# Who weighs the first token tiles, one operation for a tile's parts, an earlier first tile of a group, and four buffers for the last results

## The chip, the cores and the metric

The kernel runs on one core of a Trainium2 chip. The metric is the device time of one launch, in microseconds. The trace is one execution of the same program, taken by the hardware profiler.

## The reference

```python
q, k, v: (2, 8, 768, 64)
k_sum, v_sum = k, v by blocks of 32 rows: max, mean          # 24 per head
scores = [q k^T / 8 within a window of 16 | q k_sum^T / 8 + log 32]
x = softmax(scores) @ [v | v_sum]                            # -> (1536, 512)

noisy = x @ w_gate + log1p(exp(x @ w_noise)) * noise         # 8 experts
two best experts per token, weights = softmax of their two logits
x = sum over the two: weight * (relu(x @ w1[e]) @ w2[e])     # w1 512x1024, w2 1024x512

h = x @ w_in                                                 # 512 x 2048
out = max(0.01 h, h) @ w_out                                 # 2048 x 512
```

The change touches the last two lines and the sum over the two experts ahead of them.

## The kernel before

Three stages follow each other: attention with the gate and the sorting by expert (to 140 us), the experts (to 529 us), and the last two products, called the last stage here. Every fp32 product is made of three: both operands are split into a high part in fp32r, and a low part, what is left. For `a @ w` TensorE adds `a_hi w_hi + a_lo w_hi + a_hi w_lo`. ScalarE makes the high parts of what TensorE put out, VectorE the low parts. Each engine has its own program, and its instructions run in the order in which they are written. The engines meet at semaphores (`wait_ge`, `then_inc`).

**Picking and weighing.** The experts' outputs lie in DRAM, sorted by expert (`y_by_tile`). The 1536 tokens are 12 tiles of 128 (`NT`), in three groups (`FG`) of four (`TW`). For each tile GpSimd gathers two sets of rows, `a` and `b`, by indirect DMA (L664). Tiles 0 and 1 and all later ones land in `y_pick` (two buffers, by parity), tiles 2 and 3 in the weight buffer `stage`. Weighing makes `a = w0 a + w1 b`. GpSimd does it for tiles 0 and 1 (`combine_early`, `EARLY = 2`, three operations), VectorE for all others (`combine`, two operations, L1096 and L1098). The semaphore `combined` counts weighed tiles.

**Turning.** `turn_tokens(i, m)` on TensorE transposes tile m of group i, four 128x128 blocks, into one of two PSUM banks `f_xT_bank[m % 2]` (L1430). ScalarE's `xT_part` copies it to `f_xT_hi` in four operations of 128x128 (L822), and VectorE's `f_xT_out` makes `f_xT_lo` in four (L1105). A transpose waits until the low part of the tile two before it is done, since that frees the bank.

**Products.** The 2048 hidden features are 16 chunks (`FC`) of 128. `f_first(i, c)` makes chunk c of `h` for the group's 512 tokens: 12 matmuls of 512 columns (L1443 to L1445) into `f_h_bank[c % 2]`. Then `chunk`: ScalarE copies it (L830), VectorE takes the leaky maximum (L1113), ScalarE makes the high part (L834) and VectorE the low part (L1115). `f_second(i, c)` adds chunk c's share to the four results of the group, in four PSUM banks `f_y_bank` (L1458 to L1460), 12 matmuls. TensorE alternates `f_first(c)` and `f_second(c - 1)`. The tiles of group i + 1 are turned in the second half of group i's chunks, one ahead of every second chunk.

**Start of the stage.** For group 0 TensorE turns tiles 0 to 3. After tiles 2 and 3 it does chunks 0 and 1 for the first 256 tokens, later the other 256 tokens of each. The weights of chunks 8 to 15 come last: once all four tiles are turned, SP loads them into `stage` in eight pieces, and ScalarE (L838) and VectorE (L1131) split two of them after each of chunks 1 to 4.

**Group borders.** VectorE weighs tile 0 of the next group at the top of its loop over i, after `chunk(i, 7)`, and TensorE turns it before `f_first(i, 8)`. `group_out` copies the four results of a group to `f_y`, which has two buffers, and SP stores each (L445). The third copy waits until the store of the first has landed, also for the last group, whose copies end the kernel.

The other names: `KD` = 4, `KF` = 8 and `GT` = 512; `p01`, `p23`, `p45` and `p67` are PSUM tensors of two banks each; `xT_bank` and `y_bank` of the expert stage are in `p45` and `p67`.

Of the kernel before, what the change touches and what calls it, by code (L numbers as in the profile page):

```python
# [55 lines left out]
EARLY = 2  # L56
# [13 lines left out]
def build(nc, q, k, v, w_gate, w_noise, noise, w1, w2, w_in, w_out, out):  # L70
    ctx = ExitStack()
    with ctx:
# [148 lines left out]
        f_y_done = sem("f_y_done"); f_y_ready = sem("f_y_ready"); out_stored = [sem(f"out_stored{i}") for i in range(2)]  # L221

# [21 lines left out]
        f_xT_bank = [p23[:, DM * i:DM * (i + 1)] for i in range(2)]  # L244
        f_y_bank = [(p45, p67)[m // 2][:, DM * (m % 2):DM * (m % 2 + 1)] for m in range(TW)]
# [46 lines left out]
        def _(sp):  # L292
# [149 lines left out]
            with sp.Fori(0, NT // 2) as j:  # L442
                for r in range(2):
                    sp.wait_ge(f_y_ready, 2 * j + r + 1)
                    sp.dma_start(out[bass.ds((2 * j + r) * P, P), :], f_y[:, r, :]).then_inc(out_stored[r], 16)  # L445
            for r in range(2):
                sp.wait_ge(out_stored[r], 16 * (NT // 2 + 1))
# [3 lines left out]
        def _(pool):  # L451
# [205 lines left out]
            for i in range(NT):  # L657
                if i == TW:
                    for m in range(EARLY):
                        combine_early(m)  # L660
                if i >= TW:
                    pool.wait_ge(f_x_turned, i - 1)
                for kk in range(2):
                    pool.indirect_dma_start(out=pick_of(i, i % TW)[kk], out_offset=None, in_=ys_dram,  # L664
                                            in_offset=bass.IndirectOffsetOnAxis(ap=slots[:, kk, i:i + 1], axis=0)).then_inc(
                                                first_picked[i] if i < TW else picked[i % 2], 16)
# [3 lines left out]
        def _(act):  # L670
# [148 lines left out]
            def xT_part(i, m, par):  # L819
                act.wait_ge(f_x_turned, TW * i + m + 1)  # L820
                for c in range(KD):
                    last = nc.scalar.copy(f_xT_hi[:, group_columns(par, c, m * P, P)], f_xT_bank[m % 2][:, c * P:(c + 1) * P])  # L822
                last.then_inc(f_xT_hi_ready, 1)
# [30 lines left out]
            for c in range(KF, FC):  # L854
                chunk(FG - 1, c)


        @block.vector
        def _(dve):
# [228 lines left out]
            def combine(i, m):  # L1088

                t = TW * i + m  # L1090
                a, b = pick_of(t, m)
                if is_later(t, TW):
                    dve.wait_ge(picked[m % 2], 16 * (t - TW - m % 2 + 2))
                else:
                    dve.wait_ge(first_picked[m], 32)
                nc.vector.tensor_scalar(a, a, top_w[:, 0, bass.ds(t, 1)], None, ALU.mult).then_inc(first_term, 1)  # L1096
                dve.wait_ge(first_term, t - EARLY + 1)
                nc.vector.scalar_tensor_tensor(out=a, in0=b, scalar=top_w[:, 1, bass.ds(t, 1)], in1=a,  # L1098
                                               op0=ALU.mult, op1=ALU.add).then_inc(combined, 1)

            def f_xT_out(i, m, par):
                dve.wait_ge(f_xT_hi_ready, TW * i + m + 1)
                for c in range(KD):
                    cols = group_columns(par, c, m * P, P)
                    last = nc.vector.tensor_tensor(f_xT_lo[:, cols], f_xT_bank[m % 2][:, c * P:(c + 1) * P], f_xT_hi[:, cols].bitcast(F32), ALU.subtract)  # L1105
                last.then_inc(f_xT_lo_ready, 1)
# [10 lines left out]
            def group_out(i, first=False):  # L1117
                if first:
                    dve.wait_ge(y_stored, 16 * TILES)
# [13 lines left out]
            dve.wait_ge(combined, EARLY)  # L1133
            for m in range(EARLY, TW):
                combine(0, m)
                f_xT_out(0, m - EARLY, 0)
            for m in range(EARLY, TW):
                f_xT_out(0, m, 0)
            for c in range(KF):
                chunk(0, c)  # L1140
                for piece in last_pieces[c]:
                    last_piece(piece)
            with dve.Fori(1, FG) as i:
                combine(i, 0)
                for c in range(KF, FC):
                    m = (c - KF) // 2
                    if c % 2 == 0:
                        f_xT_out(i, m, i * -1 + 2)
# [4 lines left out]
                group_out(i - 1, True)  # L1153
                for c in range(1, KF):
                    chunk(i, c)
            for c in range(KF, FC):
                chunk(FG - 1, c)
            group_out(FG - 1)
# [3 lines left out]
        def _(pe):  # L1162
# [261 lines left out]
            def turn_tokens(i, m):  # L1424
                t = TW * i + m
                pe.wait_ge(combined, t + 1)
                if is_later(t, 2):
                    pe.wait_ge(f_xT_lo_ready, t - 1)
                for c in range(KD):
                    last = nc.tensor.transpose(f_xT_bank[m % 2][:, c * P:(c + 1) * P], pick_of(t, m)[0][:, c * P:(c + 1) * P], ident[:])  # L1430
# [35 lines left out]
            for m in range(TW):  # L1466
                turn_tokens(0, m)
                if m >= TW // 2:
                    pe.wait_ge(w1_ready, HALF_A + 1)
                    pe.wait_ge(f_xT_lo_ready, TW // 2)  # L1470
                    f_first(0, m - TW // 2, 0, 0, GT // 2)
            pe.wait_ge(f_xT_lo_ready, TW)
            for c in range(KF):
                f_first(0, c, 0, *((GT // 2, GT // 2) if c < 2 else ()))
                if c == 0:
                    pe.wait_ge(w2_ready, HALF_A + 1)
                else:
                    f_second(0, c - 1)
# [31 lines left out]
```

## Time and profile before

| | us |
|---|---|
| median of 3 runs | 812.42 (811.93 to 812.96) |
| the profiled execution | 813.08 |
| its span, first to last instruction | 811.5 |
| TensorE busy with matmuls | 771.6 (95%) |
| VectorE busy | 272.5 (34%) |
| ScalarE busy | 239.5 (30%) |
| GpSimd busy | 370.3 (46%) |
| TensorE's mean granted clock | 0.984 of full speed |

Times in the trace count from the first instruction. A row in order of time gives the start, the duration, the engine, the line of the kernel and the operation, and in brackets how long the engine had been idle and what ended this. Matmuls overlap: each lasts 0.39 us with 512 columns, while the next starts 0.23 us later. So TensorE's pace is read from start to start. PE is TensorE, DVE VectorE, ACT ScalarE, POOL GpSimd and SP the engine that issues most loads and stores.

### The profile page before, as it was taken

Reading aid. Unit: us, or ns where it says so; the run is one execution under the profiler, and the core shown is the slowest. Engines: PE = TensorE matmul, PEld = TensorE weight load, DVE = VectorE, ACT = ScalarE, POOL = GpSimd, SP = SyncE. Lnnn points to the kernel's source line nnn. Section 1 sums busy time; section 2 is a strip of 40 time slices with the busy share of each in tenths; the row PEclk is TensorE's granted clock in tenths of the full one; section 3 lists DMA queues with packets and bytes.
Section 4 is the critical chain, followed back from the end, with each engine's and each line's share of the span. In section 5 each row is a group of like instructions: output and inputs, shape, how many; then the busy total and the mean of one; then the engine's idle time right before and its main releaser. Section 6 shows DMA issues by size and latency. Waiting matters only on the chain.

```text
span 811.5 us, 12513 instructions
## 1 busy us (share of the span) xinstructions
PE 771.6 (95%) x4092; PEld 638.0 (79%) x4093; DVE 272.5 (34%) x521; ACT 239.5 (30%) x429; POOL 370.3 (46%) x317
## 2 busy tenths in 40 slices
PE   5998988799999999999999999979999999999997
PEld 4887865588888888888888888868788887888885
DVE  3776656022212212212212212256343324332223
ACT  3787555121121122122112112135232222322221
POOL 5586932568888686938478771510010001000000
PEclk9999879899999999999999999999999999999999
DMA  9959764995353625234352721353010101010001
GB/s 199 217 132 234 198 222 156 318 331 188 111 193 103 214 90 207 90 142 155 130 168 93 243 78 44 112 171 102 26 53 27 53 0 52 0 52 0 1 1 52
DMA packets 77891, 100.54 MB, mean 124 GB/s; under 512 B 46452, under 2 KB 49524, under 8 KB 77492
## 3 DMA queue, kind: packets, MB, share of 16 engines
q1 hardware_dynamic: 60164, 48.71, 21.9%
q0 software_dynamic: 12464, 43.79, 16.7%
q10 hardware_dynamic: 5232, 7.64, 2.5%
q8 instruction: 18, 0.29, 0.1%
q14 instruction: 13, 0.11, 0.0%
HBM read 78.27 MB, written 23.68 MB: 126 GB/s over the span
## 4 chain that ended last, share of the span: by engine, by line
PE 84%; DMA 4%; POOL 3%; DVE 3%; SPq 3%; issue 2%; ACT 1%; DVEq 0%; POOLq 0%; ACTq 0%
PE p L1353 42%; PE p L1443 5%; PE p L1445 5%; PE p L1444 5%; PE p L1458 5%; PE p L1460 5%; PE p L1459 5%; PE p L1345 3%; POOL stage L502 2%; PE p L1340 2%; DMA qk_other<-in_q 1%; DMA mean_rows<-v_means 1%; PE p L1308 1%; PE p L1252 1%; SPq L295 1%
## 5 line engine op out<-in xcount | busy, mean ns | idle before, releaser
L550 POOL TENSOR_TENSOR w_lo<-stage,w_hi 128x1024 fp32r<-128x1024 f32 x56 | 134.0, 2394 | 4.7
L1353 PE MATMUL p<-w_hi,xT_hi 128*128 x248 | 99.8, 402 | 1.7 <-issue 1.7
L664 POOL DMA_INDIRECT y_pick<-y_by_tile,slots x20 | 19.1, 957 | 172.5 <-PE p L1430 147.6
L1353 PE MATMUL p<-w_hi,xT_lo 128*128 x248 | 97.1, 392 | 0.0
L1353 PE MATMUL p<-w_lo,xT_hi 128*128 x248 | 97.0, 391 | 0.0
L1353 PE MATMUL p<-w_hi,hT_hi 128*128 x240 | 96.6, 402 | 0.0
L1353 PE MATMUL p<-w_lo,hT_hi 128*128 x240 | 93.9, 391 | 0.0
L1353 PE MATMUL p<-w_hi,hT_lo 128*128 x240 | 93.5, 390 | 0.0
L1443 PE MATMUL p<-f_xT_hi,w_hi 128*128 (+2 forms) x200 | 77.2, 386 | 1.7 <-DVE f_xT_lo L1105 1.7
L798 ACT CAST hT_hi<-p 128x1024 fp32r<-128x1024 f32 x30 | 30.4, 1014 | 158.0 <-PE p L1345 144.7
L1458 PE MATMUL p<-w_hi,f_hT_hi 128*128 128x512 f32 x192 | 74.9, 390 | 1.4 <-DVE f_hT_lo L1115 1.3
L1445 PE MATMUL p<-f_xT_hi,w_lo 128*128 (+2 forms) x200 | 76.2, 381 | 0.0
L1444 PE MATMUL p<-f_xT_lo,w_hi 128*128 (+2 forms) x200 | 76.2, 381 | 0.0
L1459 PE MATMUL p<-w_lo,f_hT_hi 128*128 128x512 f32 x192 | 74.7, 389 | 0.0
L1460 PE MATMUL p<-w_hi,f_hT_lo 128*128 128x512 f32 x192 | 74.7, 389 | 0.0
L1056 DVE TENSOR_TENSOR xT_lo<-p,xT_hi 128x512 fp32r<-128x512 f32 x31 | 21.4, 691 | 155.9 <-ACT xT_hi L795 149.9
L793 ACT ACTIVATE h_row<-p 128x1024 f32<-128x1024 f32 x30 | 30.8, 1026 | 142.4 <-PE p L1353 130.3
L1113 DVE SCALAR_TENSOR_TENSOR f_h<-p,f_h 128x512 f32<-128x512 f32 x48 | 33.2, 691 | 116.5 <-ACT f_h L830 116.5
L830 ACT COPY f_h<-p 128x512 f32<-128x512 f32 x48 | 28.2, 587 | 142.0 <-PE p L1445 142.0
L548 POOL TENSOR_SCALAR w_hi<-stage 128x1024 fp32r<-128x1024 f32 x56 | 59.0, 1054 | 12.1 <-DMA stage<-in_moe_w 9.4
L1062 DVE COPY y_row<-p 128x512 f32<-128x512 f32 x31 | 21.5, 692 | 116.6 <-PE p L1353 112.9
L1353 PEld LDWEIGHTS p<-w_hi,xT_hi 128*128 128x128 f32 x248 | 46.9, 189 | 11.1 <-issue 2.3
(209 smaller groups left out, 1333.1 us busy)
## 6 DMA issues: line engine op xcount, KB each, us to landing
stage<-in_moe_w POOLq DMA_DIRECT2D x48, 512.0 KB, 4.1
stage<-in_moe_w SPq DMA_DIRECT2D x16, 512.0 KB, 4.4
y_by_tile<-y_row ACTq DMA_DIRECT2D x29, 256.0 KB
x_by_tile<-x_ring SPq DMA_DIRECT2D x28, 256.0 KB
x_row<-x_by_tile SPq DMA_DIRECT2D x28, 256.0 KB
v_win<-in_v SPq DMA_DIRECT2D x8, 384.0 KB, 6.4
x_tokens<-x_out SPq DMA_DIRECT2D x12, 256.0 KB, 2.7
out<-f_y SPq DMA_DIRECT2D x12, 256.0 KB, 2.0
```

Source lines behind the costliest of these rows:

```text
L548: pool.tensor_scalar(w_hi[:, par, cols], stage[:, c % STAGES, :], 1.0, 1.0, ALU.mult, ALU.mult).then_inc(hi_split, 1)
L550: pool.tensor_tensor(w_lo[:, par, cols], stage[:, c % STAGES, :], w_hi[:, par, cols].bitcast(F32), ALU.subtract).then_inc(lo_split, 1)
L793: nc.scalar.activation(h_row[:], h_bank[:], ACT.Relu).then_inc(h_ready, 1)
L798: nc.scalar.copy(hT_hi[:].rearrange("p c m -> p (c m)"), hT_bank[:]).then_inc(hT_hi_ready, 1)
L1113: nc.vector.scalar_tensor_tensor(out=h, in0=f_h_bank[c % 2], scalar=0.01, in1=h, op0=ALU.mult, op1=ALU.max).then_inc(f_leaky_done, 1)
L1353: last = nc.tensor.matmul(bank, a, w, start=(c == 0 and i == 0), stop=(c == left_hi.shape[1] - 1 and i == 2))
L1443: nc.tensor.matmul(to, hi, f_xT_hi[:, cols], start=(k == 0), stop=False)
L1444: nc.tensor.matmul(to, hi, f_xT_lo[:, cols], start=False, stop=False)
L1445: last = nc.tensor.matmul(to, lo, f_xT_hi[:, cols], start=False, stop=(k == KD - 1))
L1458: nc.tensor.matmul(f_y_bank[m], f_hT_hi[:, c % 2, rows], hi, start=(c == 0), stop=False)
L1459: nc.tensor.matmul(f_y_bank[m], f_hT_hi[:, c % 2, rows], lo, start=False, stop=False)
L1460: last = nc.tensor.matmul(f_y_bank[m], f_hT_lo[:, c % 2, rows], hi, start=False, stop=(c == FC - 1))
```

## The change

- GpSimd weighs all four tiles of group 0, where it weighed two. `EARLY` is gone.
- A tile's high part is made in one operation of 128x512 instead of four of 128x128, and so is its low part. The output is written through a view (`turned_part`) that has the tile's columns of all four blocks.
- Tiles 2 and 3 of group 0 are turned into banks of their own, the two halves of `p45`. TensorE turns all four tiles at once, then makes chunks 0 and 1 for 256 tokens and for the other 256, then `f_first(0, 2)`, then two `f_second`, and goes on as before from chunk 3.
- Tile 0 of groups 1 and 2 is weighed by VectorE before chunk 7 of the group ahead. VectorE's loop over the groups is written out.
- The last group's four results are copied to four buffers: two halves of `f_y` and two of `y_pick`. Result 1 is copied and stored by ScalarE, the others are copied by VectorE and stored by SP.

```diff
--- before.py
+++ after.py
@@ -53,7 +53,6 @@
 TCOLS = TILES + TILES % 2
 FIRST = 3
 FULL = 2 * N // P
-EARLY = 2
 RING = 7
 ROWS = 2
 GM = TPB * 2 * E
@@ -219,6 +218,7 @@
         f_h_done = sem("f_h_done"); f_h_copied = sem("f_h_copied"); f_leaky_done = sem("f_leaky_done")
         f_hT_hi_ready = sem("f_hT_hi_ready"); f_hT_lo_ready = sem("f_hT_lo_ready"); f_chunk_done = sem("f_chunk_done")
         f_y_done = sem("f_y_done"); f_y_ready = sem("f_y_ready"); out_stored = [sem(f"out_stored{i}") for i in range(2)]
+        last_y_ready = sem("last_y_ready"); last_stored = sem("last_stored")
 
 
         q_pairs = q.rearrange("b h (t p) d -> (b h) p t d", p=P)
@@ -242,6 +242,18 @@
         last_y_bank = p67[:, DM:2 * DM]
         f_h_bank = [p01[:, GT * i:GT * (i + 1)] for i in range(2)]
         f_xT_bank = [p23[:, DM * i:DM * (i + 1)] for i in range(2)]
+        first_xT_bank = f_xT_bank + [p45[:, DM * i:DM * (i + 1)] for i in range(2)]
+        last_y = [f_y[:, 0, :], f_y[:, 1, :], y_pick[:, 0, 0, :], y_pick[:, 0, 1, :]]
+
+        def xT_bank_of(i, m):
+
+            return first_xT_bank[m] if isinstance(i, int) and i == 0 else f_xT_bank[m % 2]
+
+        def turned_part(a, par, m):
+
+            by_chunk = a[:].rearrange("p (c t) -> p c t", t=GT)
+            first = par * KD
+            return by_chunk[:, slice(first, first + KD) if isinstance(first, int) else bass.ds(first, KD), m * P:(m + 1) * P]
         f_y_bank = [(p45, p67)[m // 2][:, DM * (m % 2):DM * (m % 2 + 1)] for m in range(TW)]
 
         def weight_piece(e, c):
@@ -439,12 +451,18 @@
 
             for r in range(2):
                 sp.sem_inc(out_stored[r], 16)
-            with sp.Fori(0, NT // 2) as j:
+            with sp.Fori(0, (NT - TW) // 2) as j:
                 for r in range(2):
                     sp.wait_ge(f_y_ready, 2 * j + r + 1)
                     sp.dma_start(out[bass.ds((2 * j + r) * P, P), :], f_y[:, r, :]).then_inc(out_stored[r], 16)
+            for m in (0, 2):
+                sp.wait_ge(f_y_ready, NT - TW + m // 2 + 1)
+                sp.dma_start(out[(NT - TW + m) * P:(NT - TW + m + 1) * P, :], last_y[m]).then_inc(last_stored, 16)
+            sp.wait_ge(f_y_ready, NT - TW + 3)
+            sp.dma_start(out[(NT - 1) * P:NT * P, :], last_y[3]).then_inc(last_stored, 16)
             for r in range(2):
-                sp.wait_ge(out_stored[r], 16 * (NT // 2 + 1))
+                sp.wait_ge(out_stored[r], 16 * ((NT - TW) // 2 + 1))
+            sp.wait_ge(last_stored, 16 * TW)
 
 
         @block.gpsimd
@@ -656,7 +674,7 @@
 
             for i in range(NT):
                 if i == TW:
-                    for m in range(EARLY):
+                    for m in range(TW):
                         combine_early(m)
                 if i >= TW:
                     pool.wait_ge(f_x_turned, i - 1)
@@ -818,9 +836,7 @@
 
             def xT_part(i, m, par):
                 act.wait_ge(f_x_turned, TW * i + m + 1)
-                for c in range(KD):
-                    last = nc.scalar.copy(f_xT_hi[:, group_columns(par, c, m * P, P)], f_xT_bank[m % 2][:, c * P:(c + 1) * P])
-                last.then_inc(f_xT_hi_ready, 1)
+                nc.scalar.copy(turned_part(f_xT_hi, par, m), xT_bank_of(i, m).rearrange("p (c t) -> p c t", c=KD)).then_inc(f_xT_hi_ready, 1)
 
             def chunk(i, c):
                 n = FC * i + c
@@ -853,6 +869,12 @@
                     chunk(i, c)
             for c in range(KF, FC):
                 chunk(FG - 1, c)
+
+            act.wait_ge(f_y_done, (TW - 1) * (FG - 1) + 2)
+            act.wait_ge(out_stored[1], 16 * ((NT - TW) // 2 + 1))
+            nc.scalar.copy(last_y[1], f_y_bank[1]).then_inc(last_y_ready, 1)
+            act.wait_ge(last_y_ready, 1)
+            act.dma_start(out[(NT - 3) * P:(NT - 2) * P, :], last_y[1]).then_inc(last_stored, 16)
 
 
         @block.vector
@@ -1089,21 +1111,16 @@
 
                 t = TW * i + m
                 a, b = pick_of(t, m)
-                if is_later(t, TW):
-                    dve.wait_ge(picked[m % 2], 16 * (t - TW - m % 2 + 2))
-                else:
-                    dve.wait_ge(first_picked[m], 32)
-                nc.vector.tensor_scalar(a, a, top_w[:, 0, bass.ds(t, 1)], None, ALU.mult).then_inc(first_term, 1)
-                dve.wait_ge(first_term, t - EARLY + 1)
-                nc.vector.scalar_tensor_tensor(out=a, in0=b, scalar=top_w[:, 1, bass.ds(t, 1)], in1=a,
+                dve.wait_ge(picked[m % 2], 16 * (t - TW - m % 2 + 2))
+                nc.vector.tensor_scalar(a, a, top_w[:, 0, t:t + 1], None, ALU.mult).then_inc(first_term, 1)
+                dve.wait_ge(first_term, t - TW + 1)
+                nc.vector.scalar_tensor_tensor(out=a, in0=b, scalar=top_w[:, 1, t:t + 1], in1=a,
                                                op0=ALU.mult, op1=ALU.add).then_inc(combined, 1)
 
             def f_xT_out(i, m, par):
                 dve.wait_ge(f_xT_hi_ready, TW * i + m + 1)
-                for c in range(KD):
-                    cols = group_columns(par, c, m * P, P)
-                    last = nc.vector.tensor_tensor(f_xT_lo[:, cols], f_xT_bank[m % 2][:, c * P:(c + 1) * P], f_xT_hi[:, cols].bitcast(F32), ALU.subtract)
-                last.then_inc(f_xT_lo_ready, 1)
+                nc.vector.tensor_tensor(turned_part(f_xT_lo, par, m), xT_bank_of(i, m).rearrange("p (c t) -> p c t", c=KD),
+                                        turned_part(f_xT_hi, par, m).bitcast(F32), ALU.subtract).then_inc(f_xT_lo_ready, 1)
 
             def chunk(i, c):
 
@@ -1114,9 +1131,8 @@
                 dve.wait_ge(f_hT_hi_ready, n + 1)
                 nc.vector.tensor_tensor(f_hT_lo[:, c % 2, :], h, f_hT_hi[:, c % 2, :].bitcast(F32), ALU.subtract).then_inc(f_hT_lo_ready, 1)
 
-            def group_out(i, first=False):
-                if first:
-                    dve.wait_ge(y_stored, 16 * TILES)
+            def group_out(i):
+                dve.wait_ge(y_stored, 16 * TILES)
                 for m in range(TW):
                     if m < TW - 1:
                         dve.wait_ge(f_y_done, (TW - 1) * i + m + 1)
@@ -1130,32 +1146,38 @@
                 cols = slice(c * CW, (c + 1) * CW)
                 nc.vector.tensor_tensor(w_lo[:, 1, cols], stage[:, c % STAGES, :], w_hi[:, 1, cols].bitcast(F32), ALU.subtract).then_inc(last_lo, 1)
 
-            dve.wait_ge(combined, EARLY)
-            for m in range(EARLY, TW):
-                combine(0, m)
-                f_xT_out(0, m - EARLY, 0)
-            for m in range(EARLY, TW):
+            for m in range(TW):
                 f_xT_out(0, m, 0)
             for c in range(KF):
+                if c == KF - 1:
+                    combine(1, 0)
                 chunk(0, c)
                 for piece in last_pieces[c]:
                     last_piece(piece)
-            with dve.Fori(1, FG) as i:
-                combine(i, 0)
+            for i in range(1, FG):
                 for c in range(KF, FC):
                     m = (c - KF) // 2
                     if c % 2 == 0:
-                        f_xT_out(i, m, i * -1 + 2)
+                        f_xT_out(i, m, i % 2)
                     chunk(i - 1, c)
                     if c % 2 == 0 and m + 1 < TW:
                         combine(i, m + 1)
                 chunk(i, 0)
-                group_out(i - 1, True)
+                group_out(i - 1)
                 for c in range(1, KF):
+                    if c == KF - 1 and i + 1 < FG:
+                        combine(i + 1, 0)
                     chunk(i, c)
             for c in range(KF, FC):
                 chunk(FG - 1, c)
-            group_out(FG - 1)
+
+            for m in (0, 2):
+                dve.wait_ge(f_y_done, (TW - 1) * (FG - 1) + m + 1)
+                if m == 0:
+                    dve.wait_ge(out_stored[0], 16 * ((NT - TW) // 2 + 1))
+                nc.vector.tensor_copy(last_y[m], f_y_bank[m]).then_inc(f_y_ready, 1)
+            dve.wait_ge(f_chunk_done, FC * FG)
+            nc.vector.tensor_copy(last_y[3], f_y_bank[3]).then_inc(f_y_ready, 1)
 
 
         @block.tensor
@@ -1424,10 +1446,10 @@
             def turn_tokens(i, m):
                 t = TW * i + m
                 pe.wait_ge(combined, t + 1)
-                if is_later(t, 2):
+                if is_later(t, TW):
                     pe.wait_ge(f_xT_lo_ready, t - 1)
                 for c in range(KD):
-                    last = nc.tensor.transpose(f_xT_bank[m % 2][:, c * P:(c + 1) * P], pick_of(t, m)[0][:, c * P:(c + 1) * P], ident[:])
+                    last = nc.tensor.transpose(xT_bank_of(i, m)[:, c * P:(c + 1) * P], pick_of(t, m)[0][:, c * P:(c + 1) * P], ident[:])
                 last.then_inc(f_x_turned, 1)
 
             def f_first(i, c, par, start=0, size=GT):
@@ -1465,17 +1487,18 @@
 
             for m in range(TW):
                 turn_tokens(0, m)
-                if m >= TW // 2:
-                    pe.wait_ge(w1_ready, HALF_A + 1)
-                    pe.wait_ge(f_xT_lo_ready, TW // 2)
-                    f_first(0, m - TW // 2, 0, 0, GT // 2)
-            pe.wait_ge(f_xT_lo_ready, TW)
-            for c in range(KF):
-                f_first(0, c, 0, *((GT // 2, GT // 2) if c < 2 else ()))
-                if c == 0:
-                    pe.wait_ge(w2_ready, HALF_A + 1)
-                else:
-                    f_second(0, c - 1)
+            pe.wait_ge(w1_ready, HALF_A + 1)
+            for half in range(2):
+                pe.wait_ge(f_xT_lo_ready, TW // 2 * (half + 1))
+                for c in range(2):
+                    f_first(0, c, 0, GT // 2 * half, GT // 2)
+            f_first(0, 2, 0)
+            pe.wait_ge(w2_ready, HALF_A + 1)
+            f_second(0, 0)
+            f_second(0, 1)
+            for c in range(3, KF):
+                f_first(0, c, 0)
+                f_second(0, c - 1)
             pe.wait_ge(last_lo, CHUNKS)
             with pe.Fori(1, FG) as i:
```

## Rows read from the trace of the kernel before

**Rows 1.** Waits of TensorE, 526 to 812 us: who for whom, total, times, longest.

```profile
PE p L1430 <- DVE y_pick L1098: 3.0, 2, 1.5
PE p L1430 <- DVE f_xT_lo L1105: 2.0, 1, 2.0
PE p L1443 <- DVE f_xT_lo L1105: 1.7, 2, 1.3
PE p L1458 <- DVE f_hT_lo L1115: 1.3, 1, 1.3
```

**Rows 2.** TensorE in order of time: start, us, what, idle before.

```profile
529.52 1.03 PE L1430 MATMUL p<-ident,y_pick 128*128 128x128 f32 x8
...
534.51 0.36 PE L1443 MATMUL p<-f_xT_hi,w_hi 128*128 128x256 f32 x1 [1.35 <-DVE f_xT_lo L1105]
...
536.01 0.60 PE L1430 MATMUL p<-ident,stage 128*128 128x128 f32 x4
...
542.87 0.50 PE L1458 MATMUL p<-w_hi,f_hT_hi 128*128 128x512 f32 x1 [1.34 <-DVE f_hT_lo L1115]
...
551.16 0.39 PE L1443 MATMUL p<-f_xT_hi,w_hi 128*128 128x512 f32 x1
```

**Rows 3.** ScalarE in order of time, start of the last stage.

```profile
530.15 1.45 ACT L822 CAST f_xT_hi<-p 128x128 fp32r<-128x128 f32 x8 [7.77 <-PE p L1430]
...
540.13 0.59 ACT L830 COPY f_h<-p 128x512 f32<-128x512 f32 x1 [2.71 <-PE p L1445]
...
543.97 1.99 ACT L838 CAST w_hi<-stage 128x1024 fp32r<-128x1024 f32 x2
```

**Rows 4.** VectorE in order of time, start of the last stage.

```profile
540.75 0.69 DVE L1113 SCALAR_TENSOR_TENSOR f_h<-p,f_h 128x512 f32<-128x512 f32 x1 [2.42 <-ACT f_h L830]
...
545.05 2.36 DVE L1131 TENSOR_TENSOR w_lo<-stage,w_hi 128x1024 fp32r<-128x1024 f32 x2 [0.26 <-ACT w_hi L838]
```

**Rows 5.** All engines in order of time, the tail.

```profile
804.54 1.39 DVE L1126 COPY f_y<-p 128x512 f32<-128x512 f32 x2 [1.05 <-PE p L1460]
...
806.17 0.39 PE L1460 MATMUL p<-w_hi,f_hT_lo 128*128 128x512 f32 x1
807.49 1.39 DVE L1126 COPY f_y<-p 128x512 f32<-128x512 f32 x2 [1.56 <-DMA out<-f_y]
```

**Rows 6.** GpSimd and VectorE in order of time, end of the expert stage.

```profile
515.42 1.29 POOL L655 TENSOR_TENSOR y_pick<-y_pick 128x512 f32<-128x512 f32 x1
...
516.00 1.23 DVE L1056 TENSOR_TENSOR hT_lo<-p,hT_hi 128x1024 fp32r<-128x1024 f32 x1 [3.19 <-ACT hT_hi L798]
...
518.79 1.29 POOL L655 TENSOR_TENSOR y_pick<-y_pick 128x512 f32<-128x512 f32 x1
...
522.42 1.22 DVE L1056 TENSOR_TENSOR last_hT_lo<-p,last_hT_hi 128x1024 fp32r<-128x1024 f32 x1 [5.19 <-ACT last_hT_hi L816]
```

**Rows 7.** The tile `stage`, 526 to 565 us: landing of the transfers into it.

```profile
DMA to landing us min/median/max: 3.2/4.8/10.5
```

**Rows 8.** In order of time, the first tiles of group 1.

```profile
576.46 0.69 DVE L1113 SCALAR_TENSOR_TENSOR f_h<-p,f_h 128x512 f32<-128x512 f32 x1 [3.37 <-ACT f_h L830]
...
578.13 0.39 PE L1460 MATMUL p<-w_hi,f_hT_lo 128*128 128x512 f32 x1
...
580.39 0.48 PE L1443 MATMUL p<-f_xT_hi,w_hi 128*128 x1
...
591.18 0.39 PE L1460 MATMUL p<-w_hi,f_hT_lo 128*128 128x512 f32 x1
...
591.77 0.48 PE L1443 MATMUL p<-f_xT_hi,w_hi 128*128 x1
```

**Rows 9.** DMA queues and stores, 655 to 760 us: packets, MB, share of 16 engines.

```profile
q0 software_dynamic: 320, 1.05, 3.6%
q1 hardware_dynamic: 576, 1.05, 2.6%
...
out<-f_y SPq DMA_DIRECT2D x4, 256.0 KB, 2.0
```

## The prediction

> **What bounds the kernel now.** I first read the busy times and the waits of TensorE after the expert stage. The table above has TensorE busy for 771.6 of 811.5 us, so only its idle stretches can be won. From 250 us to the end of the expert stage it waits for nobody; after that four rows hold all its waits, 8.0 us [rows 1]: 3.0 us, twice, for VectorE to weigh a group's first tile, and 2.0, 1.7 and 1.3 us at the start of the last stage. Then I read TensorE's order of time there [rows 2]: the transposes of tiles 0 and 1 start at 529.52, the first product of the stage at 534.51, and the first `f_second` at 542.87. At 551.16 `f_first(0, 3)` starts and the flow is steady. What it waited for stands in ScalarE's and VectorE's order of time [rows 3, 4]. VectorE weighs tiles 2 and 3 between the low parts of tiles 0 and 1, so all four arrive late. The last part I read is the tail [rows 5]: the last product starts at 806.17 and the span ends at 811.5. In between VectorE copies four results through two buffers, and the third copy, 807.49, waited 1.56 us for the store of the first to land.
>
> **Term A, the start of the stage.** Removed from VectorE: two weighings, each a `tensor_scalar` and a `scalar_tensor_tensor`. Added to GpSimd: two of its own, three operations each. In [rows 6] the add of tile 0 starts at 515.42 and that of tile 1 at 518.79, so a weighing takes 3.37 us. The four end at 518.79 + 1.29 + 2 x 3.37 = 526.8, before TensorE comes to tile 0 at 529.52, and tile 3 is asked for only 12 transposes later. Cover 2.7 us or more: cost nothing.
> The gathers for tiles 4 and 5 stand behind the weighings on GpSimd, but they also wait for the transposes of tiles 2 and 3, which now come earlier, and their data is wanted at 573 us.
>
> Tile 3 no longer waits for a bank, since tiles 2 and 3 get `p45`. The 16 transposes run at about 0.11 us each (eight in 1.03) from 529.52 to 531.3. ScalarE makes a high part in one operation. No row has this one with an output in four pieces. The nearest is the 128x512 copy from the same memory, 0.59 [rows 3]; the upper bound is four operations as now, eight of which took 1.45 (0.72 for a tile). VectorE's low part in one operation is bounded by 0.69 [rows 4] and by 0.9, the four operations now. Nothing here lets either fall below the nearest row. I take 0.59 and 0.69: size and memories are the same. High part 0 starts at 530.15 as now and ends 530.74, high part 1 ends 531.3. VectorE is free of `y_row` at 530.4, so low part 0 runs 530.77 to 531.46 and low part 1 ends at 532.07 (back to back a start follows 0.08 before the end of the one before). Low part 3 ends at 533.3.
>
> TensorE starts `f_first(0, 0)` at 532.13 instead of 534.51. Its four half products are 12 matmuls each, 1.50 us (534.51 to 536.01), together 5.9, so they end at 538.0, and low part 3 was there long before. The first chunk's sum is complete at 536.7. ScalarE's copy (0.59) and VectorE's leaky step (0.69) end at 538.05, and `f_first(0, 2)`, which needs that bank, starts at 538.11, a stall of 0.1. It takes 2.8, and the two `f_second` 2.72 each: `f_first(0, 3)` starts at 546.37. That compares with 551.16: **A = 4.8 us**. By the upper bounds of the one-operation parts it is 4.3.
>
> What is queued behind: chunk 1's low part ends at 541.4. Then ScalarE splits two pieces of the last weights (1.99) and VectorE follows (2.36), so chunk 2's leaky step starts at 544.0 and its low part is ready at 546.0. TensorE asks for it at 546.37 + 2.72 = 549.1, 3 us later. The piece loads leave SP's queue when tile 3 is turned, at 531.4 instead of 536.7. The transfers into `stage` landed within 10.5 us [rows 7], so by 542.4; ScalarE can use them from 540.5, and the delay that this could give, 1.9, lies within the 3.
>
> The Trainium skill, "Perfetto Trace Analysis", section "Optimizing Scalar/DVE Operations", speaks against this step: GpSimd and VectorE share a read port of SBUF, so that moving operations between them "might not help". The trace does not show it for the operations that stand beside the weighing. A low part of VectorE at 516.00 overlaps GpSimd's add of 515.42 and takes 1.23 us, against 1.22 for the same operation alone at 522.42 [rows 6]. If the port did hold `last_hT_lo` back by one GpSimd operation, A would be up to 1 us less.
>
> **Term B, a group's first tile.** VectorE now weighs it ahead of chunk 7. Its picks landed tens of us before, and VectorE idles 3.37 us ahead of that chunk's leaky step [rows 8]. Now matmul, weighing, transposes stand in a row: 578.13 to 580.39 between the last product and the next one. At tile 5, whose weighing is not late, the same two matmuls lie 591.18 to 591.77 apart [rows 8]. So 2.26 - 0.59 = 1.67 each, and by the same reading 1.73 at the second border: **B = 3.4 us**. The bounds are 0 (if something else holds TensorE there) and 3.4. I take the upper one, since it is the weighing that ended both waits [rows 1]. Unrolling VectorE's loop and the weighing's new place cost nothing: chunk 7's leaky step still comes 2 us after the weighing ends.
>
> The Trainium skill, "Runtime: NRT & Kernel Launch", section "Instruction fetch mechanics", says that a taken branch to code outside the fetched window stops the engine until it is fetched. At TensorE's branch back, 669 us, this would leave a part of the second 1.7 us. The trace speaks against it: from 655 to 760 us only data queues moved anything [rows 9].
>
> **Term C, the tail.** Result 0 is copied at 804.54 as now, result 1 by ScalarE, result 2 when its sum is ready at 805.9 (until 806.6), and result 3, whose last product starts at 806.17 and takes 0.39, from 806.6 to 807.3. In the kernel before, the last of the four copies ended at 807.49 + 1.39 = 808.88 [rows 5]. Behind it lie an issue and a store that landed 2.0 us later [rows 9], and they stay. Four stores will start within 2.1 us instead of 4. Four such stores in the middle of the stage, 1.05 MB, took 2.6% of 105 us [rows 9], 0.68 each, about as fast as they will be issued: at most 0.2 us is lost. **C = 1.6 less 0.1 = 1.5 us**, bounds 1.4 and 1.6.
>
> **Sum.** 4.8 + 3.4 + 1.5 = 9.7. The profiled execution took 813.08 (span 811.5) and becomes 803.4. The median of the runs is 0.66 below it, so the forecast is **812.42 - 9.7 = 802.7 us**.
>
> **Rivals.**
> 1. *The start is won, its second half not.* Chunk 2 stands behind the weight pieces on ScalarE and VectorE. If these come later than by my margin of 3 us, `f_second(0, 2)` waits, and of A only the earlier start, 534.51 - 532.13 = 2.4, is left. That gives 802.7 + 2.4 = 805.1. For it: GpSimd's gathers and SP's loads now start together. Against it: the margin. Chance 0.10.
> 2. *The earlier weighing doesn't do what it is for*, because TensorE is held at a group's border by its own loop. B = 0, 806.1. What ended the waits [rows 1] and the queues without instruction fetches [rows 9] speak against it. Chance 0.06.
> 3. *The tail's stores queue*, or the parts take the upper bounds: 0.5 to 1.5 us less, 803.2 to 804.2. Chance 0.12.
> 4. *Slower: GpSimd becomes what the stage waits for.* Tile 3 is asked for at 530.8 and weighed at 526.8, so each us of delay beyond 4 costs one. For the kernel to be slower than before it must be over 13.7 us late: two weighings of 10.2 instead of 3.37. They run beside two VectorE operations only. Chance 0.02.
>
> The forecast has 0.70. A change that this measurement can tell from none is about 0.2%, 1.6 us. Rivals 1 to 3 are all faster by more than that, so faster 0.95, same 0.03 (several of them at once), slower 0.02. The forecast's own range is 802.0 to 803.7; taking in rival 3 and rival 1, it is 801.8 to 805.2.
>
> **What would show it.** Right: no wait of TensorE on a weighing any more; the first product of the stage 2.4 us or so sooner after the first transpose (2.6 instead of 5.0); `f_first(0, 3)` 16.9 us after it instead of 21.6; 0.6 between the matmuls around each group's first transposes; the last copy ending 1.5 us sooner after the last product. Wrong: a one-operation part over 0.8 us, a wait of `f_second(0, 2)` on `f_hT_lo`, an idle TensorE at 573 or 664 us, or a last store that lands more than 2.2 us after its issue.

## The result, and the profile after

| | before | changed |
|---|---|---|
| median of 4 runs each, us | 812.69 | 800.54 (799.66 to 802.11) |
| profiled execution, us | 813.08 | 802.11 |
| its span, us | 811.5 | 800.7 |
| TensorE busy, us | 771.6 | 767.8 |

The ratio is 0.9858, with a 95% interval of 0.9828 to 0.9887: 9 to 14 us faster. The forecast was 802.7, with a range from 801.8. The kernel is faster than the range allows. The forecast gain of 9.7 us still lies inside the interval of this one comparison, near its lower end; the further comparisons below narrow that down.

Waits of TensorE after the expert stage, in the changed kernel (who for whom, total us, times, longest):

```profile
PE p L1465 <- DVE f_xT_lo L1122: 0.8, 1, 0.8
PE p L1465 <- DVE f_h L1130: 0.2, 1, 0.2
```

Of the 8.0 us of [rows 1] 1.0 is left, and the waits on a weighing are gone. TensorE in order of time, start of the last stage:

```profile
528.00 1.03 PE L1452 MATMUL p<-ident,y_pick 128*128 128x128 f32 x8
528.87 1.04 PE L1452 MATMUL p<-ident,stage 128*128 128x128 f32 x8
530.69 0.35 PE L1465 MATMUL p<-f_xT_hi,w_hi 128*128 128x256 f32 x1 [0.78 <-DVE f_xT_lo L1122]
...
536.39 0.28 PE L1467 MATMUL p<-f_xT_hi,w_lo 128*128 128x256 f32 x1
536.91 0.50 PE L1465 MATMUL p<-f_xT_hi,w_hi 128*128 128x512 f32 x1 [0.24 <-DVE f_h L1130]
...
539.76 0.39 PE L1480 MATMUL p<-w_hi,f_hT_hi 128*128 128x512 f32 x1
...
545.20 0.39 PE L1465 MATMUL p<-f_xT_hi,w_hi 128*128 128x512 f32 x1
```

The first product comes 2.69 us after the first transpose (4.99 before), `f_first(0, 3)` 17.20 us (21.64 in [rows 2]). ScalarE and VectorE there:

```profile
528.63 2.05 ACT L839 CAST f_xT_hi<-p 128x512 fp32r<-128x512 f32 x4 [7.71 <-PE p L1452]
535.55 0.59 ACT L846 COPY f_h<-p 128x512 f32<-128x512 f32 x1 [4.86 <-PE p L1467]
...
539.40 2.00 ACT L854 CAST w_hi<-stage 128x1024 fp32r<-128x1024 f32 x2
...
529.25 2.49 DVE L1122 TENSOR_TENSOR f_xT_lo<-p,f_xT_hi 128x512 fp32r<-128x512 f32 x4 [0.36 <-ACT f_xT_hi L839]
536.16 0.69 DVE L1130 SCALAR_TENSOR_TENSOR f_h<-p,f_h 128x512 f32<-128x512 f32 x1 [4.42 <-ACT f_h L846]
...
540.48 2.36 DVE L1147 TENSOR_TENSOR w_lo<-stage,w_hi 128x1024 fp32r<-128x1024 f32 x2 [0.26 <-ACT w_hi L854]
```

Four high parts in 2.05 us and four low parts in 2.49, back to back. So a part in one operation costs what the nearest rows had, 0.60 and 0.69. ScalarE's copy at 535.55 came 0.3 us after the sum was complete; this delay stands in this trace alone, and is the 0.2 us wait on `f_h`. GpSimd in order of time:

```profile
524.09 1.29 POOL L673 TENSOR_TENSOR stage<-stage 128x512 f32<-128x512 f32 x1
529.75 0.98 POOL L682 DMA_INDIRECT y_pick<-y_by_tile,slots  x1 [4.36 <-PE p L1452]
```

The last weighing ends at 525.4, 2.6 us ahead of the first transpose, and the gathers behind it start once the transposes of tile 2 are done. A group border, on TensorE:

```profile
572.17 0.39 PE L1482 MATMUL p<-w_hi,f_hT_lo 128*128 128x512 f32 x1
572.41 0.60 PE L1452 MATMUL p<-ident,y_pick 128*128 128x128 f32 x4
572.76 0.48 PE L1465 MATMUL p<-f_xT_hi,w_hi 128*128 x1
```

From the last product to the next one 0.59 us, 2.26 in [rows 8]. The tail, all engines:

```profile
795.26 0.69 DVE L1178 COPY f_y<-p 128x512 f32<-128x512 f32 x1 [1.07 <-PE p L1482]
...
795.96 0.59 ACT L875 COPY f_y<-p 128x512 f32<-128x512 f32 x1 [2.49 <-PE p L1482]
...
796.57 0.35 ACTq L877 DMA_DIRECT2D out<-f_y  x1
796.65 0.69 DVE L1178 COPY y_pick<-p 128x512 f32<-128x512 f32 x1 [0.70 <-PE p L1482]
...
796.91 0.39 PE L1482 MATMUL p<-w_hi,f_hT_lo 128*128 128x512 f32 x1
797.34 0.69 DVE L1180 COPY y_pick<-p 128x512 f32<-128x512 f32 x1
...
798.06 0.33 SPq L462 DMA_DIRECT2D out<-y_pick  x1
```

The last copy ends at 798.03, 1.12 us after the start of the last product, against 2.71 in [rows 5].

Three stretches give the terms, each from mark to mark. The marks are the first transpose of the last stage, the start of `f_first(0, 3)`, VectorE's first copy of the last group, and the end of the span.

| us | before | changed | gained | forecast |
|---|---|---|---|---|
| ahead of the first transpose | 529.52 | 528.00 | 1.52 | 0 |
| A, to `f_first(0, 3)` | 21.64 | 17.20 | 4.44 | 4.8 |
| B, to the first last copy | 253.38 | 250.06 | 3.32 | 3.4 |
| C, to the end | 6.96 | 5.44 | 1.52 | 1.5 |
| span | 811.5 | 800.7 | 10.8 | 9.7 |

The parts gained 9.3 us, a little less than forecast. The surprise lies elsewhere: 1.5 us in stages that the change doesn't touch, and a gain of the medians (12.15 us) that is larger by another 1.3. Part of it is busy time: TensorE was busy for 3.8 us less in the changed kernel, though it does the same products, and 3.1 of these lie in the first 150 us (126.1 against 123.0 us busy), where the granted clock was 0.94 before and 0.96 after.

### The profile page after: what moved, and what is told of

Same layout as the page of the kernel before. It is cut to its first block, busy times and chain, and to the rows that moved or that the text cites. A ratio compares the mean times of both kernels' runs of the same rounds, so it can differ in the third digit from the quotient of the medians.

```text
span 800.7 us, 12291 instructions
## 1 busy us (share of the span) xinstructions
PE 767.8 (96%) x4092; PEld 636.1 (79%) x4093; DVE 267.3 (33%) x480; ACT 237.7 (30%) x394; POOL 377.5 (47%) x323
## 4 chain that ended last, share of the span: by engine, by line
PE 90%; DVE 3%; DMA 2%; issue 2%; ACT 2%; SPq 1%; DVEq 0%; ACTq 0%
PE p L1375 43%; PE p L1465 5%; PE p L1467 5%; PE p L1466 5%; PE p L1480 5%; PE p L1482 5%; PE p L1481 5%; PE p L1367 4%; PE p L1215 2%; PE p L1362 2%; PE p L1330 1%; PE p L1243 1%; DMA qk_nat<-in_q 1%; PE p L1274 1%; DMA qk_other<-in_q 1%
## 5 line engine op out<-in xcount | busy, mean ns | idle before, releaser
L1084 DVE COPY y_row<-p 128x512 f32<-128x512 f32 x31 | 21.5, 692 | 114.9 <-PE p L1375 114.9
```

## The experiments

Each comparison below has its own runs of the kernel before, on one chip, and different comparisons ran on different chips. So a ratio is always taken within one comparison.

**The same kernels again** (e1 and e2, nothing edited).

> The changed kernel once more, nothing edited. In its first trace the three parts of the change gained 9.3 us (4.4 at the start of the last stage, 3.3 at the two group borders, 1.5 in the tail), and the first transpose of the last stage came at 528.00 instead of 529.52, 1.5 us sooner, in stages that the change doesn't touch. Theory 1, chance: this lead varies from execution to execution, the kernel gains 9.3 us on average (803.4 against 812.7), and in this trace the first transpose lies anywhere between 527.5 and 530.5. Theory 2, systematic: something in the changed program (two more semaphores, other program lengths) makes the earlier stages faster; the first transpose is again 1.5 us or more sooner than in the kernel before, and the gain is 11 to 13 us.

> The kernel before, nothing edited, timed against itself. Theory 1: its first transpose of the last stage moves by 1 us or more from 529.52, to either side, and its time lies within 0.2% of 812.7. Theory 2: the first transpose stays within 0.4 us of 529.5. Both: ratio 1.000 within 0.002.

Measured for e1: ratio 0.9838 (0.9806 to 0.9869), 795.3 us. For e2: ratio 1.0003 (0.9977 to 1.0029). The runs of the kernel before spread from 802.0 to 811.6 us here; the three that the prediction started from had spread from 811.93 to 812.96. The first transposes came at 523.39 (e1) and 520.90 (e2), so what lies ahead of the last stage varies by many us in both kernels, and a lead of 1.5 means nothing. That much of theory 1 held, though not its sizes: it had the first transpose of e1 between 527.5 and 530.5, and the time of e2 within 0.2% of 812.7, where the median was 808.0. And the gain, 13 us, was over theory 1's 9.3. The second trace of the kernel before shows what the first did not have. From the first transpose to the first last copy it takes 276.65 us, not 275.02, with nearly the same waits. Busy time and clock by window, the first 22 us of the last stage (busy us, matmuls, granted clock, DMA share, GB/s), first in the old trace of the kernel before, then in the new one:

```profile
529.52:551.52 22.00, 16.98 (x103) 1.00 0.62 203
```

```profile
520.90:542.90 22.00, 17.75 (x96) 0.84 0.57 190
```

In smaller windows of the new one:

```profile
521.00:525.00 4.00, 1.98 (x13) 0.87 0.17 66
525.00:527.00 2.00, 1.11 (x5) 0.50 0.06 8
527.00:529.00 2.00, 2.00 (x11) 0.50 0.73 193
529.00:531.00 2.00, 2.00 (x12) 0.55 0.29 90
531.00:533.00 2.00, 2.00 (x19) 1.00 0.92 250
```

And the matmuls there in order of time:

```profile
520.90 1.03 PE L1430 MATMUL p<-ident,y_pick 128*128 128x128 f32 x8
523.91 1.04 PE L1430 MATMUL p<-ident,stage 128*128 128x128 f32 x4 [1.98 <-DVE f_xT_lo L1105]
525.88 0.55 PE L1443 MATMUL p<-f_xT_hi,w_hi 128*128 128x256 f32 x1 [0.93 <-DVE f_xT_lo L1105]
526.24 0.41 PE L1444 MATMUL p<-f_xT_lo,w_hi 128*128 128x256 f32 x1
526.45 0.41 PE L1445 MATMUL p<-f_xT_hi,w_lo 128*128 128x256 f32 x1
```

The granted clock falls to 0.50, the lower of TensorE's two levels (1.2 of 2.4 GHz), at the end of the wait of 1.98 us: four transposes now take 1.04 us. In the old trace they took 0.63 (at 532.53), behind the same wait of 1.98. The clock stays low until about 530.5. Matmuls of 256 columns then follow each other by 0.21 us instead of 0.12. The Trainium skill, "TensorE: Matmul & The Clock Gate", section "What's actually happening", says that idling throttles this clock and activity releases it; these rows agree.

**One part at a time** (e3 to e6, each from the kernel before).

```diff
 e3: everything of the change except the next two
 e4: VectorE's loop written out, combine(i, 0) gone from its top, and
+                if c == KF - 1:
+                    combine(1, 0)
...
+                    if c == KF - 1 and i + 1 < FG:
+                        combine(i + 1, 0)
 e5: the four buffers, ScalarE's copy and store of result 1
 e6: VectorE's loop written out only
-            with dve.Fori(1, FG) as i:
+            for i in range(1, FG):
```

> The start of the last stage alone (GpSimd weighs all four tiles, one operation for a tile's parts, four banks, the new order on TensorE); group borders and tail as before. From the first transpose to f_first(0, 3): 17.2 us instead of 21.6, as in the changed kernel. Group borders and tail as before. Theory 1: gain 4.4 us, 808.2. Theory 2: 4.4 plus 1.5 to 3 if the cause lies in the programs of GpSimd or ScalarE, which this kernel shares with the changed one.

> The earlier weighing of a group's first tile alone, with VectorE's loop written out. TensorE's two waits of 1.5 us at the group borders vanish, and 0.6 us lie between the matmuls around the transposes there. Theory 1: gain 3.3 us, 809.4. Theory 2: 3.3 plus 1.5 to 3, if the cause lies in VectorE's program, which is written out here as in the changed kernel.

> The four buffers for the last results alone (two more semaphores, ScalarE copies and stores result 1). From VectorE's first copy of the last group to the end of the span 5.4 us instead of 7.0, so the gain is 1.5 us, 811.2, by theory 1 (the lead ahead of the last stage is chance). By theory 2 (systematic) and if the cause lies in the two more semaphores or in SP's program: 3 to 4.5 us.

> VectorE's loop over the groups written out, nothing else. Theory 1: no difference, 812.7 within 0.2%, and TensorE's waits as in the kernel before. Theory 2, if the cause lies in VectorE's program length: 1.5 to 3 us faster, with the first transpose of the last stage at 528 or sooner.

| | ratio to before | gain, us | clock, first 22 us | from first transpose to first last copy | from there to the end |
|---|---|---|---|---|---|
| e3, start | 0.9918 (0.9890 to 0.9946) | 6.6 | 1.00 | 270.30 | 6.98 |
| e4, sooner | 0.9947 (0.9918 to 0.9976) | 4.3 | 0.92 | 273.16 | 6.97 |
| e5, buffers | 0.9980 (0.9946 to 1.0014) | 1.6 | 0.92 | 276.26 | 5.41 |
| e6, unrolled | 1.0000 (0.9971 to 1.0028) | 0.0 | 0.84 | 276.63 | 6.93 |

e5 alone is within the noise by its time; its tail, 5.41 us against 6.95, is the gain of 1.5. e6 rules out the length of VectorE's program as a cause. Waits of TensorE in e4:

```profile
PE p L1433 <- DVE f_xT_lo L1105: 2.0, 1, 2.0
PE p L1446 <- DVE f_xT_lo L1105: 1.7, 2, 1.3
PE p L1461 <- DVE f_hT_lo L1115: 1.3, 1, 1.3
```

The waits of the start are those of [rows 1], and both waits on a weighing are gone. e3 alone has the clock at 1.00, and gained about 2 us more than the 4.4 that its waits explain, which is what theory 2 had said. But the surplus doesn't lie ahead of the last stage: its transposes came at 520.6, where those of e6 with the old start came at 519.8. From the first transpose to the first last copy it takes 6.35 us less than e2, and that is nearly all of the 6.6.

**Parts of the start taken back** (e7 and e8, from the changed kernel; the lines shown are the main ones).

```diff
 e7, and the same for the low part:
-                nc.scalar.copy(turned_part(f_xT_hi, par, m), ...)
+                for c in range(KD):
+                    last = nc.scalar.copy(f_xT_hi[:, group_columns(par, c, m * P, P)], ...)
 e8:
-                    for m in range(TW):
+                    for m in range(2):
                         combine_early(m)
...
+            for m in range(2, TW):
+                combine(0, m)
+                f_xT_out(0, m - 2, 0)
```

> The changed kernel with a tile's high and low part made in four operations each, as before. My prediction's bounds make the one-operation parts worth 0.45 us at the start of the stage; rival: more, since VectorE runs four such parts one behind the other (4 x 0.2 = 0.8). First product 3.1 us instead of 2.7 after the first transpose. Time 0.4 to 0.8 us above the changed kernel; group borders as in the changed kernel.

> The changed kernel, but VectorE weighs tiles 2 and 3, between the low parts, as before. The weighing of a tile takes VectorE 1.2 us, two of them lie ahead of low part 1, so the first product comes 2 us later (4.7 instead of 2.7 after the first transpose) and the kernel is 2.0 us slower than the changed one. Rival: less than 1 us, because ScalarE's parts were what set the start and VectorE had room.

Ratios to the kernel before: e7 0.9862 (0.9817 to 0.9908), e8 0.9877 (0.9834 to 0.9919). The times can't tell them from the changed kernel; the traces can. From the first transpose to the first last copy e7 takes 267.53 us and e8 268.94, where four further traces of the changed kernel have 266.97 to 267.02. So one operation per part is worth 0.5 us, and the weighing on GpSimd 1.9. TensorE's wait in e8:

```profile
PE p L1459 <- DVE stage L1120: 2.2, 2, 1.1
```

With 2.2 us of waits in two pieces the clock stayed at 1.00 in e8's trace.

**The clock, both ways** (e9 fills the waits of the kernel before, e10 makes one longer in the changed kernel).

```diff
 e9:
+            def keep_busy(count):
+                for _ in range(count):
+                    nc.tensor.matmul(p45[:, DM:2 * DM], w_hi[:, 0, 0:P], w_hi[:, 0, 0:DM], start=True, stop=True)
+            pe.wait_ge(w1_ready, HALF_A + 1)
                 turn_tokens(0, m)
+                if m == 1:
+                    keep_busy(8)
+                if m == 2:
+                    keep_busy(6)
...
+                    if c == 1:
+                        keep_busy(6)
                     f_second(0, c - 1)
 e10, on VectorE ahead of f_xT_out(0, 0, 0):
+            for _ in range(4):
+                link(nc.vector.tensor_copy(f_xT_lo[:, KD * GT:KD * GT + GT], p67[:, DM:2 * DM]))
```

> The kernel before with TensorE kept busy in its waits at the start of the last stage: 8 matmuls of 512 columns without use after the transposes of tile 1, 6 after tile 2, and 6 ahead of f_second(0, 0). Every wait stays, TensorE's idle time there falls from 5 us to about 1. Four of the five traces with the old start show a granted clock of 0.84 to 0.92 over the first 22 us of the last stage, with rows of 256 columns 0.21 us apart instead of 0.12, and the five with the new start show 1.00. Theory 1, the clock falls because TensorE idles in this stretch: here the mean clock of those 22 us is 1.00, and from the first transpose to the first copy of the last group it takes 275.0 to 275.6 us instead of the 276.3 to 276.6 of the traces with the fall; time 0.5 to 1.5 us below the kernel before. Theory 2, the clock has another cause (the transfers in this stretch, the place in the program): it is below 1.00 here too, and the time is 0 to 1 us above the kernel before.

> The changed kernel with VectorE held for 3.5 us (four copies without use, one after the other) ahead of the first low part, so that TensorE idles some 4.3 us at one place at the start of the last stage. Theory 1 (idling lets the clock fall): the granted clock there is below 1.00 in this trace, and the kernel loses 3.5 us plus 1 to 2. Theory 2: clock 1.00, loss 3.5 us.

e9, the first 22 us of the last stage, and TensorE's waits:

```profile
522.38:544.38 22.00, 21.50 (x123) 1.00 0.61 203
```

```profile
PE p L1430 <- DVE y_pick L1098: 3.0, 2, 1.5
PE p L1443 <- DVE f_xT_lo L1105: 0.3, 1, 0.3
```

TensorE is busy for 21.5 of 22 us (17.0 before), its work is no sooner done, and the clock is 1.00. From the first transpose to the first last copy it takes 275.00 us, as the one trace of the kernel before that had no fall (275.02), and 1.3 to 1.7 less than the others. The time, ratio 0.9981 (0.9944 to 1.0017), is 1.5 us lower, which the noise covers. e10, TensorE in order of time, and the first 22 us:

```profile
521.76 1.04 PE L1454 MATMUL p<-ident,stage 128*128 128x128 f32 x8
526.02 0.55 PE L1467 MATMUL p<-f_xT_hi,w_hi 128*128 128x256 f32 x1 [3.22 <-DVE f_xT_lo L1122]
526.37 0.41 PE L1468 MATMUL p<-f_xT_lo,w_hi 128*128 128x256 f32 x1
526.58 0.41 PE L1469 MATMUL p<-f_xT_hi,w_lo 128*128 128x256 f32 x1
```

```profile
520.89:542.89 22.00, 18.78 (x107) 0.92 0.59 203
```

VectorE's copies ran in part beside the transposes, so the longest wait grew only from 0.8 to 3.2 us. By the end of this wait the clock is low, rows 0.21 apart. The stretch to the first last copy takes 270.69 us, 3.7 more than in the changed kernel: 2.4 of longer wait, and 1.3 of clock. Ratio 0.9898 (0.9857 to 0.9939). Theory 1 held in both directions. Each direction rests on one trace, and the kernel before had one without a fall as well, so e9 alone could be luck. That none of the traces with the new start but e10 shows a fall is the stronger sign.

**More traces and times** (nothing edited).

> The kernel before once more, for its trace. Theory 1: like the second trace, 0.84 to 0.92 over the first 22 us of the last stage, 276.3 to 276.6 us from the first transpose to the first copy of the last group; 1.00 and 275.0 as in the first trace in the fewer cases.

> The changed kernel once more, for its trace. Theory 1: clock 1.00 over the first 22 us of the last stage, and 267.0 to 267.3 us from the first transpose to the first copy of the last group. Both theories: what lies ahead of the first transpose differs by several us from the other traces of the same kernel.

> The changed kernel again. Theory 1 (the rest is chance): gain 10.6 us, ratio 0.987, clock 1.00 over the first 22 us of the last stage and 267.0 to 267.3 us from the first transpose to the first copy of the last group. Theory 2 (a real lead ahead of the last stage): gain 12 us or more, ratio 0.985 or less, first transpose sooner on average than in the traces of the kernel before.

> The same once more, for a narrower interval. Theory 1: ratio 0.987. Theory 2: ratio 0.985 or less.

> The kernel before against itself, as the measure of what the comparison can tell: ratio 1.000, with an interval of 0.3% to either side. Its trace: a fall of the clock in the first 22 us of the last stage (0.84 to 0.92) and 276.3 to 276.6 us to the first copy of the last group, in most cases.

| | ratio | first transpose | clock, first 22 us | to the first last copy | to the end |
|---|---|---|---|---|---|
| before | | 529.52 | 1.00 | 275.02 | 6.96 |
| e2 | 1.0003 | 520.90 | 0.84 | 276.65 | 6.95 |
| e11 | | 526.06 | 0.92 | 276.46 | 6.98 |
| e15 | 1.0002 (0.9983 to 1.0021) | 521.02 | 0.92 | 276.55 | 6.93 |
| changed | 0.9858 | 528.00 | 1.00 | 267.26 | 5.44 |
| e1 | 0.9838 | 523.39 | 1.00 | 266.99 | 5.42 |
| e12 | | 523.31 | 1.00 | 266.97 | 5.42 |
| e13 | 0.9867 (0.9845 to 0.9889) | 518.64 | 1.00 | 267.02 | 5.44 |
| e14 | 0.9858 (0.9831 to 0.9886) | 521.96 | 1.00 | 267.02 | 5.42 |

Over all kernels the clock fell in six of the seven traces with the old start (not in the very first) and in none of the eight with the new one, e9 and e10 not counted. Only in e2 did it fall at the first wait. In the other five it fell during the second, of 1.35 us, or up to 0.2 us behind it, as in e15, where the first product takes 0.55 us instead of the 0.36 of [rows 2]:

```profile
524.04 0.63 PE L1430 MATMUL p<-ident,stage 128*128 128x128 f32 x4 [1.98 <-DVE f_xT_lo L1105]
526.01 0.55 PE L1443 MATMUL p<-f_xT_hi,w_hi 128*128 128x256 f32 x1 [1.35 <-DVE f_xT_lo L1105]
```

From the first transpose to the end the kernel before takes 283.1 us on average (four traces), the changed one 272.5 (five): 10.6 us. The four ratios average 0.9855, 11.7 us of 808. The 1.1 us between the two is no more than the intervals of the ratios allow by chance. The first transpose comes 1.3 us sooner on average in the changed kernel, with a spread of 9 us within either kernel. So a small lead ahead of the last stage is neither shown nor excluded.

The mean clock of whole executions points the same way. Over the experiments, on four chips, it averages 0.988 in 110 executions of the kernel before and 0.991 in 19 of the changed one. At an equal mean clock the changed kernel is 9.7 us shorter, both at 0.989 (805.4 against 795.7; 20 and 3 executions) and at 0.991 (804.2 against 794.6; 10 and 4). On average over all it is 11.8 us shorter. So some 2 us of the gain go with the clock. A part of that lies ahead of the last stage, and nothing shows that the change caused that part.

## Why the prediction was wrong

**What bounds the kernel.** The reading held: TensorE's idle stretches, the four rows of waits, the tail. The sentence that "only its idle stretches can be won" is the step that failed. An idle stretch at the start of the last stage also slows what follows it, since the clock then mostly falls to half, for 3.5 to 7 us by the mean clocks of 0.92 and 0.84 over 22 us. In three of the four traces of the kernel before this cost 1.4 to 1.6 us between the same marks (276.46 to 276.65 against 275.02), 1.2 on average over the four. Removing the waits gives that back too. No term stood for it, and the trace that the sum was made against was the one without a fall. How often the clock fell in the runs of the first comparison can't be told: its one trace of the kernel before shows no fall.

**Term A** was right. Start to start it measured 4.4 us in the first trace and 4.7 in e1 (540.33 less 523.39 is 16.94, against 21.64) for a forecast of 4.8; the 0.3 us is ScalarE's late copy. The one-operation parts cost what the nearest rows had (0.60 and 0.69), GpSimd's weighings ended 2.6 us early for a forecast of 2.7, and `f_second(0, 2)` waited for nothing. The shared port of which the prediction warned shows no cost: VectorE's low part at 520.96 took 1.22 us beside GpSimd's add of 520.72, as it did alone in [rows 6].

**Term B** was right: 3.32 for 3.4. So rival 2 did not occur. The second border, at the branch back of TensorE's loop, has 0.58 us between the matmuls (661.25 to 661.83), as the first has 0.59, so the branch costs nothing that shows.

**Term C** was right: 1.52 for 1.5. Rivals 1, 3 and 4 did not occur.

**From the sum to the time.** The forecast took the spread of three runs (0.13%) for what a measurement can tell. Later runs of the same kernel spread over 10 us, because what lies ahead of the last stage varies. The four comparisons put the gain at 11.7 us; the sum of 9.7 plus the clock's 1.2 makes 10.9, and the marks of nine traces give 10.6. So a range that ended 0.9 us below the forecast was too narrow on the side on which a term was missing. What stands between 10.9 and the 12.15 of the first medians is within their interval. The marks alone would have put the time at the end of the range, so that the first medians lie 1.3 us outside it is in part chance.

## What to carry to other kernels

Price an idle stretch of TensorE twice: once as the wait itself, and once as the clock that may be at half behind it, which one trace can fail to show. Take more than one trace of the kernel before, and sum within a stage from mark to mark: with the clock alike, those stretches repeated within 0.3 us, while whole spans spread over 10. The weighing that moved to an idle engine was free here, because it ended 2.6 us before it was wanted. Of the 4.7 us of the start it was worth 1.9 (e8) and the one-operation parts 0.5 (e7). The 2.3 left go to the new order on TensorE and the two more banks, by subtraction; no run takes these back alone.

## What the runs showed of the hardware

- TensorE's granted clock fell to 0.50 at the end of an idle piece of 1.98 us (e2), at one of 1.35 us that followed one of 1.98 us, or up to 0.2 us behind it (five traces), and in one of 3.2 us (e10). It did not fall at the lone 1.5 us of a group border, nor in e8 with 1.09 and 1.12 us. The same program showed it in one execution and not in another: of the four traces of the kernel before three have it, and the first, with waits of 1.98 and 1.35 us, has not.
- Executions of one kernel differ by 10 us, and the mean granted clock goes with it. Of twelve in e2 the fastest, 801.99 us, had a mean clock of 0.993 and the slowest, 811.61, one of 0.981; 0.012 of 805 us is 9.7 us. From TensorE's first transposes of `x_row` to the last stage all nine traces of the two kernels took 355.4 to 356.1 us at a clock of 1.00. The difference lies ahead of that mark, which came between 163.2 and 174.1 us, with a clock of 0.93 to 0.98 there. Why it differs is open.
- A copy of 128x512 whose output lies in four pieces takes what one in a single piece does: 0.60 us on ScalarE, 0.69 on VectorE.
